# Scoring and transposing attention tiles two at a time on one Trainium2 core

## What is computed

```
scores = q @ k.T / sqrt(D) + bias[head]            # 576 x 576 for each (batch, head)
attn   = softmax(scores)                           # exp, row sums + 1e-9
x      = (attn @ v), heads side by side            # 2304 tokens x 512
x      = (h * cos(h)) @ w_out,  h = x @ w_in       # 512 -> 2048 -> 512
y      = (silu(xn @ w_gate) * (xn @ w_val)) @ w_out2, xn = rmsnorm(x)   # 512 -> 1536 -> 512
```

## Time and profile before

| | |
|---|---|
| time, median of 3 runs (lowest to highest) | 1208.93 us (1208.05 to 1209.38) |
| profiled execution, its time | 1208.74 us |
| profiled execution, span from first to last instruction | 1207.0 us |
| mean granted TensorE clock | 0.996 of full |
| TensorE busy | 1171.1 us, 97% |
| VectorE / ScalarE / GpSimd busy | 58% / 41% / 41% |
| attention on TensorE | 68 to 341 us |

### The profile page before, as it was taken

One profiled execution on the slowest core, in us unless ns is written; L12 is line 12 of the kernel. 1 busy time (PEld: TensorE's weight loads), 2 busy tenths in 40 slices (PEclk: granted clock), 3 DMA queues, 4 the chain that ended last, 5 costly groups with the idle time before them and its releaser, 6 DMA issues. The chain is left out here.

```text
span 1207.0 us, 21829 instructions
## 1 busy us (share of the span) xinstructions
PE 1171.1 (97%) x7464; PEld 1078.6 (89%) x7464; DVE 704.4 (58%) x1540; ACT 496.3 (41%) x1034; POOL 490.4 (41%) x515
## 2 busy tenths in 40 slices
PE   5789999999989999999999999999999999999998
PEld 2267777777779999999999999999999999999998
DVE  8978888888889867777786887553011020210201
ACT  6967787787723433333343333111111111111111
POOL 3047777777766342525243362751111111111111
PEclk9989999999999999999999999999999999999999
DMA  5754535252144000000000011330000000000000
GB/s 172 247 174 126 170 99 170 100 188 81 56 114 123 18 2 1 0 0 0 0 0 0 0 36 35 105 114 27 1 1 26 0 26 0 0 26 0 26 0 26
DMA packets 46534, 69.06 MB, mean 57 GB/s; under 512 B 3712, under 2 KB 27424, under 8 KB 46496
## 3 DMA queue, kind: packets, MB, share of 16 engines
q1 hardware_dynamic: 46496, 68.60, 18.3%
HBM read 53.25 MB, written 15.34 MB: 57 GB/s over the span
## 5 line engine op out<-in xcount | busy, mean ns | idle before, releaser
L820 PE MATMUL banks<-x_high,w_low_rest 128*128 128x384 f32 x672 | 224.5, 334 | 0.0
L818 PE MATMUL banks<-x_high,w_high_rest 128*128 128x384 f32 x672 | 224.4, 334 | 0.0
L819 PE MATMUL banks<-x_low,w_high_rest 128*128 128x384 f32 x672 | 224.4, 334 | 0.0
L1367 DVE TENSOR_TENSOR X<-X,banks 128x384 f32<-128x384 f32 x72 | 39.8, 552 | 298.6 <-PE banks L820 298.5
L1386 POOL TENSOR_TENSOR product_low<-X,product_high 128x384 fp32r<-128x384 f32 x72 | 72.8, 1012 | 345.5 <-ACT product_high L1329 345.5
L1184 POOL TENSOR_TENSOR product_low<-g,product_high 128x384 fp32r<-128x384 f32 x96 | 102.3, 1066 | 236.9 <-ACT product_high L1066 236.9
L818 PE MATMUL bank<-product_high,w_high_rest 128*128 128x384 f32 x480 | 162.1, 338 | 0.8 <-POOL product_low L1184 0.8
L820 PE MATMUL bank<-product_high,w_low_rest 128*128 128x384 f32 x480 | 160.5, 334 | 0.0
L819 PE MATMUL bank<-product_low,w_high_rest 128*128 128x384 f32 x480 | 160.5, 334 | 0.0
L1094 ACT ACTIVATE angle<-angle,quarter 128x384 f32<-128x384 f32 x96 | 59.3, 617 | 201.9 <-DVE angle L1126 201.9
L644 DVE CUSTOM_DVE_ANT_0 probs<-banks,bias 128x576 f32<-128x576 f32 (+1 forms) x160 | 119.7, 748 | 20.6 <-PE banks L506 10.0
(11 more groups left out here) (113 smaller groups left out, 2525.4 us busy)
## 6 DMA issues: line engine op xcount, KB each, us to landing
raw_qk<-in_qk SPq DMA_DIRECT2D x32, 576.0 KB, 3.8
bias_scratch<-bias_stage SPq DMA_DIRECT2D x36, 288.0 KB, 3.2
bias<-bias_scratch SPq DMA_DIRECT2D x32, 288.0 KB, 3.4
w_raw<-in_w_out SPq DMA_DIRECT2D x28, 256.0 KB, 2.7
values<-in_v SPq DMA_DIRECT2D x16, 320.0 KB, 4.1
w_raw<-in_w_in SPq DMA_DIRECT2D x16, 256.0 KB, 2.9
out_t<-X SPq DMA_DIRECT2D x5, 768.0 KB, 3.6
w_raw<-in_w_gate SPq DMA_DIRECT2D x12, 256.0 KB, 3.3
```

The source lines that it names most:

```text
L818: nc.tensor.matmul(out, high, x_high, start=start, stop=False)
L819: nc.tensor.matmul(out, high, x_low, start=False, stop=False)
L820: return nc.tensor.matmul(out, low, x_high, start=False, stop=stop)
```

## The change

The loops of the attention phase now step by two tiles. On TensorE `slot` becomes `slots`: score(s), score(s + 1), then the two sets of transposes, then one piece of the mix. The pieces move from slots 3, 5, 8, 0 to 4, 6, 8, 0. On VectorE two tiles are handled per step as well: add_bias(s), guard and invert of s - 1, add_bias(s + 1), normalise(s - 2), guard and invert of s; `keep_end` moves to the step of slot 4, `keep_mixed` to that of slot 6. The lists of ScalarE, POOL and SyncE stay. No instruction is added or removed, apart from register instructions and waits.

```
-MIX_SLOTS = (3, 5, 8, 0)
+MIX_SLOTS = (4, 6, 8, 0)
...
-            def slot(n, parity, s, step, compute=True):
+            def slots(n, parity, s, step, compute=True):
                 if compute:
                     score(n, s, step == 0)
-                if s < T_LAG:
-                    if step > 0:
-                        turn(n - 1, TILES - T_LAG + s, False)
-                elif compute:
-                    turn(n, s - T_LAG, step == 0)
+                    score(n, s + 1, step == 0)
+                for r in (s, s + 1):
+                    if r < T_LAG:
+                        if step > 0:
+                            turn(n - 1, TILES - T_LAG + r, False)
+                    elif compute:
+                        turn(n, r - T_LAG, step == 0)
...
-                for s in range(TILES):
-                    slot(n, parity, s, step)
+                for s in range(0, TILES, 2):
+                    slots(n, parity, s, step)
...
+            def sum_inverse(n, parity, step, s):
+                m, _, r = back(n, parity, s, EXP_LAG)
+                if s >= EXP_LAG or step > 0:
+                    guard(m, r)
+                    invert(m, r)
+
             def pair(n, parity, step, hp=None):
-                for s in range(TILES):
-                    m, _, r = back(n, parity, s, EXP_LAG)
-                    m3, _, r3 = back(n, parity, s, EXP_LAG + 1)
+                for s in range(0, TILES, 2):
+                    m2, _, r2 = back(n, parity, s, EXP_LAG + 1)
                     if hp is not None:
                         dve.wait_ge(att.bias_in[s], (hp + 1) * 16)
                     add_bias(n, s, step == 0)
-                    if s >= EXP_LAG or step > 0:
-                        guard(m, r)
-                    if (s >= EXP_LAG + 1 or step > 0) and r3 not in POOL_TILES:
-                        normalise(dve, m3, r3, dve_normed)
-                    if s >= EXP_LAG or step > 0:
-                        invert(m, r)
-                    if step > 0 and s == T_LAG - 1:
+                    sum_inverse(n, parity, step, s)
+                    if hp is not None:
+                        dve.wait_ge(att.bias_in[s + 1], (hp + 1) * 16)
+                    add_bias(n, s + 1, step == 0)
+                    if s >= EXP_LAG + 1 or step > 0:
+                        normalise(dve, m2, r2, dve_normed)
+                    sum_inverse(n, parity, step, s + 1)
+                    if step > 0 and s == T_LAG:
                         keep_end(n - 1, 1 - parity)
```

More of the change, by code:

```diff
@@ L580, in _ @@
                 pair(m * 2 + 1, 1, 2)
-            for s in range(MIX_SLOTS[1] + 1):
-                slot(PAIRS, 0, s, 2, compute=False)
+            for s in range(0, MIX_SLOTS[1] + 1, 2):
+                slots(PAIRS, 0, s, 2, compute=False)
             pe.wait_ge(biased, PAIRS * TILES)
```

## The result

The changed kernel takes 1216.16 us (median of 4, 1215.94 to 1216.86) against 1208.49 us before on the same chip (median of 4, 1207.51 to 1209.38): ratio 1.0068, 95% interval 1.0056 to 1.0080.

A forecast was written before the change was run, and what follows sets the result against it. TensorE, busy 97% and never waiting in the steady state, was taken as the bound; 6.0 us of seams, 2.2 of waits and 0.6 at the end, 8.8 on 1208.74, gave 1217.5 us, range 1212.5 to 1222.

The forecast's parts named there:

- account of a pair: TensorE, steady state: work 14.6 us plus 1.64 of shape-switch losses makes 16.3 a pair, with no waiting for other engines.
- price of alternation: TensorE: switching between scores and full transposes costs nothing, so doing them in twos gains 0.
- The rival on the other side of no change: TensorE: each alternation costs 0.08 us, so fewer save 6.4 us; extra returns cost nothing; 1205 us, chance of faster 0.06.
- The main term: TensorE: 64-row transposes parted from mixes cost 0.40 us more a pair in shape switches, 6.0 us, bounds 3 and 9.
- The waits: TensorE before tile 0's transposes waits for VectorE's normalise in slots 2 and 3: 0.15 a pair, 2.2 us, bounds 0 and 12.
- near tie: Slots 2 and 3: VectorE's second add, needed by tile 5's score, is over only when that score comes, 2.95 against 3.0.
- VectorE's own work: VectorE: guard and invert back to back add about 0.1 us a step, covered by its free 2.3 us in 16: 0.
- Start 0 and end 0.6: Pairs 0 and 1 taken as 0, within 1 us; a later mix copy delays the cos layer's first matmul by 0.6 us.
- The ring as the bound: VectorE and ScalarE become the bound; wait before tile 0's transposes grows to 0.8 us; 1227 us, chance 0.12 (1222 and up).
- The new seams partly hidden: TensorE: score or full-transpose weights load during the short 64-row set; seams cost only 3.0 us; 1213 us, chance 0.10.
- nothing: Whole kernel: saved start-ups and new shape-switch losses cancel, no measurable change, 1209 to 1211 us, chance 0.06.

The follow-up runs named there:

- half undone within pairing: Changed kernel with the mix directly behind tile 4's 64-row transposes, ahead of tile 5's full ones: 1213.16 us, ratio 1.0047 against the kernel before.
- all three edits together: Changed kernel with mix at slot 2, mix directly behind tile 4's 64-row transposes, and VectorE's two adds before guard and invert: 1211.94 us, ratio 1.0035.

## Why the prediction was right, point by point

- **The account of a pair and the price of alternation.** Right, but for pairs 8 and 12 of before: there tile 3's score starts 0.12 late, with the first distance of 0.24 that a wait leaves, which is the 0.14 named above. The single-tile kernel with the mix moved costs 0.39 by seams alone. The change costs 0.36 of seams and 0.20 of wait and load by its own rows, which is all of its 0.57. For five fewer alternations between scores and transposes in a pair nothing is left over, so they were free. The rival on the other side of no change needed 0.08 for each, 0.40 a pair, and is out.
- **The main term, seams at 0.40 a pair.** Right as a mechanism, shown twice: made without pairing, and half undone within pairing (-0.19). Its size was 0.36, since the return from 64 rows to transposes costs 0.15 and not 0.20. The Trainium skill's "TensorEngine Tiling", under Key Properties, has a change of tiling mode drain TensorE; the trace agrees for the return that no row had shown before, at 314.21 to 314.38. It gives no price, and the price depends on what comes next.
- **The waits, 0.15 a pair.** The size was nearly right (0.20 with the load that it exposes, 0.1 without), which was luck, since the place and the step behind it were wrong. I put the second add 0.92 behind the first, by the row in which a copy follows the reciprocal, and took the transposes of tile 8 as the bound (2.15 into the step). The kernel with both adds first bears that bound out (2.16), but it does not come last. An add behind guard and reciprocal comes 1.14 after the last add, and this case was in the trace of before, in VectorE's timeline:

```profile
297.05 0.76 DVE L644 CUSTOM_DVE_ANT_0 probs<-banks,bias 128x576 f32<-128x576 f32 x1
...
298.19 0.76 DVE L644 CUSTOM_DVE_ANT_0 probs<-banks,bias 128x576 f32<-128x576 f32 x1
```

The changed kernel has the same distance, and it decides:

```profile
304.29 0.76 DVE L646 CUSTOM_DVE_ANT_0 probs<-banks,bias 128x576 f32<-128x576 f32 x1
...
305.44 0.76 DVE L646 CUSTOM_DVE_ANT_0 probs<-banks,bias 128x576 f32<-128x576 f32 x1
...
306.12 0.52 DVE L412 TENSOR_SCALAR probs<-probs,inv_total 128x576 f32<-128x576 f32 x1
```

  The step began at 303.16. The first add stands at 1.13 (forecast 1.12), the second at 2.28 (forecast 2.15), and tile 5's score 0.82 behind that, at 3.10, where it was due at 3.00. The near tie that I had written down for it (2.95 against 3.0) was the one that broke. Tile 0's normalise then took 0.52 and not the mean of 0.77, so it was done at 3.48 and its transposes did not wait. A mean over all normalises was the wrong row for one at a known place (its length goes with what POOL runs, as told at the end).
- **VectorE's own work, 0.** Right in sum, since nothing new waits for VectorE outside this step.
- **Start 0 and end 0.6.** Start: the first score came 0.40 earlier and pairs 0 and 1 grew by 0.04, where the forecast had pair 1 grow by 0.55. End: pair 15 with the end was forecast at 0.55 + 0.6 = 1.15 and measured at 0.53. With 7.07 against 13 x 0.55 = 7.15 for pairs 2 to 14, these make the 1.6 us between forecast and profiled times. That the median came within 1.3 us of the forecast says little about these two terms. Rows of the end: TensorE's first matmul of the cos layer in the changed kernel, then VectorE's `keep_end` before and after:

```profile
340.57 0.41 PE L825 MATMUL banks<-x_high,w_high_head 128*128 128x384 f32 x1 [0.43 <-DVE x_low L819]
```

```profile
329.86 0.69 DVE L661 COPY probs_t_end<-bank 128x512 f32<-128x512 f32 x1 [0.63 <-PE bank L532]
...
336.95 0.69 DVE L663 COPY probs_t_end<-bank 128x512 f32<-128x512 f32 x1
```

  The copy of the last mix but two does come later, 20.21 after pair 15's first score instead of 19.28. But before, VectorE waited 0.63 behind it for transposes before it could run `keep_end`, and the changed kernel has no wait there (336.95). So `keep_end` is later by 0.39 alone, x_low by 0.54 (23.28 instead of 22.74 behind pair 15's first score), and the first matmul of the cos layer is not later at all (24.38 instead of 24.52, and it waits 0.43 instead of 0.73). The last mix, behind the four x_low, ends 0.53 later. The step that the forecast left out is this slack of 0.63: a term of 0.6 was added where pair 15's own 0.55 was all that came through.
- **The ring as the bound.** Out for the change, where the wait is 0.1 plus an exposed load. But waits for VectorE and POOL are near: the runs with VectorE's list changed alone, with the mix in one piece, and with both adds first each found some.
- **The new seams partly hidden.** Out: 0.36 of the 0.40 is there, and the single-tile kernel with the mix moved shows it in clean rows. The change is clear of noise, so "nothing" is out too.

## What to carry to other kernels

When one engine is full and its records follow each other without a gap, sum its work by starts and list what is lost; if the only loss is seams between shapes, an order that is neater in another way can only be judged by the seams it adds. Instructions of two smaller shapes belong next to each other, so that one return serves both. In a tight step take each distance from a row with the same neighbours on the engine, not from a mean or from a row with another successor, and ask of each result that is moved later who waits for it, for that is where the wait goes.

## What was unexpected in the hardware

**A late release costs more than its wait.** Where a paired step's second score waits for a semaphore, its weight load is late too, and the first distance is 0.23 or 0.24 instead of 0.13. So each wait of 0.09 to 0.41 there cost 0.10 or 0.11 on top. It holds even when the wait itself is too short to see: the full 0.11 in pairs 2 and 3 of the changed kernel, 0.08 with both adds first, and 0.06 with all three edits together.

**A normalise on VectorE has several lengths.** Durations of line 412 on DVE from 97 to 325 us (ns, least, median, most), in the kernel before and in the changed one:

```profile
L412 DVE TENSOR_SCALAR probs<-probs,inv_total x71: 501/652/1604, 96.4 to 324.7; 128x576 f32<-128x576 f32 x57, 64x576 f32<-64x576 f32 x14
```

```profile
L412 DVE TENSOR_SCALAR probs<-probs,inv_total x68: 505/516/842, 96.2 to 323.0; 128x576 f32<-128x576 f32 x55, 64x576 f32<-64x576 f32 x13
```

The same operation moved behind another instruction became a fifth shorter in the median. The traces show what its length goes with: what POOL runs as it begins. In the kernel before, 14 of these normalises began with POOL idle and took 0.50 or 0.51. Another 29 began during POOL's TENSOR_TENSOR of line 351 or 357; they took 0.54 to 1.60 and ended 0.31 or 0.32 after POOL's instruction did, like this one (POOL, then VectorE):

```profile
197.38 1.42 POOL L351 TENSOR_TENSOR k_low<-raw_qk,k_high 128x576 fp32r<-128x576 f32 x1
```

```profile
197.56 1.55 DVE L412 TENSOR_SCALAR probs<-probs,inv_total 128x576 f32<-128x576 f32 x1
```

Of the 25 that began during POOL's TENSOR_SCALAR of line 347, 14 took 0.50 all the same, and 11 took 0.63 to 0.74 and ended 0.31 after it. In the changed kernel 54 of 67 began during a normalise of POOL's own and ended 0.31 to 0.37 after it, most of them near its end, hence 0.52. The 1.44 of the earlier trace rows had begun during a TENSOR_TENSOR of POOL as well. No run moved POOL's list, so this is an observation in the traces and not a tested cause.

**The clock at the end of attention.** In the run of the change again, behind three waits for x_low like those of the first profile (0.45, 0.70 and 0.76; there 0.43, 0.70 and 0.76), the granted clock fell from 1.00 (2.4 GHz) to 0.50 (1.2 GHz) between 346 and 348, and was 1.00 again from 349 on. A window (busy us of PE, PEld, DVE, ACT and POOL, then the mean granted clock) and the timeline of that run:

```profile
346.00:351.00 5.00, 4.30 (x19) 1.93 (x18) 0.46 (x1) 0.00 (x0) 0.88 (x1) 0.71 0.32 95
```

```profile
346.07 3.55 PE L546 MATMUL bank<-probs_t,values 128*64 128x288 f32 x16
```

In the first profile of the change the clock is 1.00 from 345 to 350.

The mix of 16 records took 3.55 instead of 2.16, and from the cos layer's first matmul to the last record of the last mix it took 8.67 instead of 7.05. That is 1.6 of the 2.3 us between the two profiled executions of the changed kernel. The kernel with both adds first fell too (0.66 from 347 to 352). The wait of 0.70 in the middle stands in six of the twelve profiled executions, and in two of these the clock fell. In the six without it (as before, where the stretch takes 6.39) it did not. What decides between these is open.
